# Attention and a feed-forward layer on one core: how the inverse row sums get from one column to all partitions

## The reference

```python
# q, k, v: (4, 8, 1152, 64) fp32; w_in (512, 2048), w_out (2048, 512), alpha (2048)
q_pool = q.reshape(B, H, S // 2, 2, D).mean(axis=3)            # 576 queries per head
scores = scale * np.matmul(q_pool, k.transpose(0, 1, 3, 2))
scores = scores - np.max(scores, axis=-1, keepdims=True)
attn = np.exp(scores)
attn = attn / (np.sum(attn, axis=-1, keepdims=True) + 1e-09)
attn_out = np.matmul(attn, v)
x = attn_out.transpose(0, 2, 1, 3).reshape(2304, 512)
h = x @ w_in
g = np.maximum(h, 0.0) + alpha * np.minimum(h, 0.0)
return g @ w_out
```

## Time and profile before

| | |
|---|---|
| median of three runs | 931.14 us (930.97 to 931.58) |
| profiled execution, own time | 932.26 us |
| its span, first to last instruction | 929.7 us |
| TensorE busy | 95% of the span |
| VectorE busy | 56% |
| ScalarE busy | 46% |
| GpSimd busy | 23% |
| mean granted TensorE clock | 0.998 of full speed |
| one row maximum (L432) | 1348 ns |
| one long exponential (L348) | 1112 ns |
| one copy of slot 1 (L465) | 692 ns |

### The profile page before, as it was taken

How to read it: one execution, slowest core, us unless ns; L and a number is a source line. 1 busy time by engine, 2 the same in 40 slices (tenths; PEclk the granted TensorE clock), 3 DMA queues, 4 the chain that set the end, 5 groups by cost and what they waited for, 6 DMA issues and landing times. The chain is left out here.

```text
span 929.7 us, 20770 instructions
## 1 busy us (share of the span) xinstructions
PE 887.3 (95%) x6896; PEld 623.2 (67%) x6896; DVE 516.9 (56%) x836; ACT 423.4 (46%) x963; POOL 213.3 (23%) x182
## 2 busy tenths in 40 slices
PE   3799999999999999999999999999999999999997
PEld 1455555555555555555545799989999999989995
DVE  2676767677767776767676344344444444343442
ACT  2566666666666666666666222222322222322222
POOL 2112111211121112111200323323232323323230
PEclk9999999999999999999999999999999999999999
DMA  7435423542354235523520122212422222322211
GB/s 186 106 83 135 119 65 82 133 121 63 82 133 123 60 82 133 127 57 82 133 71 1 59 68 58 67 62 63 136 57 68 57 68 61 132 59 66 65 36 68
DMA packets 36366, 79.57 MB, mean 86 GB/s; under 512 B 5360, under 2 KB 9456, under 8 KB 36336
## 3 DMA queue, kind: packets, MB, share of 16 engines
q1 hardware_dynamic: 33936, 74.48, 31.0%
q10 hardware_dynamic: 2400, 4.72, 1.5%
HBM read 74.46 MB, written 4.72 MB: 85 GB/s over the span
## 5 line engine op out<-in xcount | busy, mean ns | idle before, releaser
L432 DVE TENSOR_REDUCE neg_max<-s_ps 128x1 f32<-128x1152 f32 x144 | 194.1, 1348 | 16.6 <-DVEq L431 16.6
L573 PE MATMUL pv_ps<-pt,v_f 128*64 128x256 f32 (+1 forms) x1152 | 169.0, 414 | 0.0
L532 PE MATMUL s_ps<-k_f,q_f 64*128 64x512 f32 (+1 forms) x640 | 160.2, 626 | 5.2 <-PEq L543 5.2
L348 ACT ACTIVATE e_sb<-s_ps,neg_max 128x1024 f32<-128x1024 f32 x144 | 160.1, 1112 | 0.0
L587 PEld LDWEIGHTS slot_ps<-ident,e_sb 64*128 64x128 f32 x2304 | 86.0, 139 | 82.4 <-issue 82.4
L465 DVE COPY pt<-slot_ps 128x512 f32<-128x512 f32 x144 | 99.6, 692 | 61.3 <-DVEq L464 59.4
L341 ACT ACTIVATE e_sb<-s_ps,neg_max 128x128 f32<-128x128 f32 x144 | 52.9, 367 | 171.5 <-ACTq L340 171.5
L617 PE MATMUL slot_ps<-x_hi,wi_hi 128*128 128x384 f32 x384 | 129.5, 337 | 1.1 <-PEq L613 1.1
L617 PE MATMUL slot_ps<-x_lo,wi_hi 128*128 128x384 f32 x384 | 129.5, 337 | 0.0
L617 PE MATMUL slot_ps<-x_hi,wi_lo 128*128 128x384 f32 x384 | 129.0, 336 | 0.0
L479 DVE TENSOR_SCALAR e_sb<-slot_ps,alpha_sb 128x384 f32<-128x384 f32 x96 | 59.3, 618 | 123.2 <-DVEq L477 123.2
(11 more groups left out here) (46 smaller groups left out, 1098.8 us busy)
## 6 DMA issues: line engine op xcount, KB each, us to landing
q_raw<-in_q SPq DMA_DIRECT2D x64, 288.0 KB, 4.5
k_f<-in_k SPq DMA_DIRECT2D x64, 288.0 KB, 4.2
wi_raw<-in_w_in SPq DMA_DIRECT2D x48, 256.0 KB, 2.6
wo_raw<-in_w_out SPq DMA_DIRECT2D x48, 256.0 KB, 2.6
v_f<-in_v SPq DMA_DIRECT2D x32, 288.0 KB, 3.0
out<-pt ACTq DMA_DIRECT2D x6, 768.0 KB, 4.4
k_end<-in_k SPq DMA_DIRECT2D x64, 32.0 KB, 4.0
alpha_sb<-in_alpha SPq DMA_DIRECT2D x1, 8.0 KB, 4.7
```

What stands on the lines that cost most here:

```text
L348: nc.scalar.activation(e_sb[:, b * NKEY + at:b * NKEY + at + n], s_ps[:, S_AT[b] + at:S_AT[b] + at + n], ACT.Exp, bias=neg_max[:, b:b + 1] ...
L432: nc.vector.tensor_reduce(out=neg_max[:, b:b + 1], in_=s_ps[:, S_AT[b]:S_AT[b] + NKEY], op=ALU.max, axis=AX_X, negate=True).then_inc(max_r ...
L532: ins = nc.tensor.matmul(s_ps[to:to + m, S_AT[b] + at:S_AT[b] + at + BANK], q_f[2 * g + h][rows, first:first + m], k_f[2 * g + h][rows, at ...
L573: ins = nc.tensor.matmul(pv_ps[h * D:(h + 1) * D, 0:n], v_f[2 * g + h][:, a, :], pt[:, a, at:at + n], start=(a == 0), stop=(a == KT - 1))
```

## The change

The matmuls of `spread_inverse` and ScalarE's copies into `inv_bc` go, on all engines; so do the waits for slot 0 in steps t = 6 and t = 1. Instead SP writes each column of inverses to a row `sums` in DRAM, 128 single elements per DMA (64 for the halves of the mixed tile): six stores for group 0, four for group 1. It waits until all have landed and reads the row back twice, once per head, broadcast to 64 partitions of `inv_bc`. `inv_bc` has room for both groups now. `scale` waits for the two broadcasts in place of ScalarE's copy. SP's loads are split into q with k, and V, to make room for the spreads in its order: group 0 goes ahead of the V loads, group 1 behind the second q, and the first weights stand between the last two spreads.

```diff
+            def load_qk_pair(pair, g):
                 load_q(pair * 2)
                 sp.wait_ge(k_free[g], 1).then_inc(k_free[g], -1)
                 load_k(pair * 2, 2 * g), load_k(pair * 2 + 1, 2 * g + 1)
                 load_q(pair * 2 + 1)
+
+            def load_v_pair(pair, g):
                 sp.wait_ge(v_free[g], 1).then_inc(v_free[g], -1)
                 load_v(pair * 2, 2 * g), load_v(pair * 2 + 1, 2 * g + 1)
+
+            def spread(group):
+                a, b = GROUP_TILES[group]
+                at, other, n, first = GROUPS[group]
+                whole = [t for t in range(a, b) if t != MIX]
+                sp.wait_ge(inv_ready, 1).then_inc(inv_ready, -1)
+                for i in range(0, len(whole), 2):
+                    for h in range(2):
+                        to = GROUPS[group][h] + i // 2 * P
+                        t = whole[i + h]
+                        sp.dma_start(sums[to:to + P], inv_sum[:, t:t + 1]).then_inc(inv_stored, 16)
+                if group == 0:
+                    for h in range(2):
+                        to = GROUPS[group][h] + 2 * P
+                        sp.dma_start(sums[to:to + HALF],
+                                     inv_sum[h * HALF:(h + 1) * HALF, MIX:MIX + 1]).then_inc(inv_stored, 16)
+                stores = len(whole) + (2 if group == 0 else 0)
+                sp.wait_ge(inv_stored, 16 * stores).then_inc(inv_stored, -16 * stores)
+                for h in range(2):
+                    row = sums[GROUPS[group][h]:GROUPS[group][h] + n]
+                    sp.dma_start(inv_bc[h * D:(h + 1) * D, first:first + n],
+                                 row.rearrange("(o n) -> o n", o=1).to_broadcast([D, n])).then_inc(inv_bc_in[group], 16)
...
+            spread(0)
+            load_qk_pair(2, 0)
+            spread(1)
+            with sp.Fori(0, NPAIR // 2 - 2) as two:
                 for g in range(2):
-                    load_pair(two * 2 + g, g)
+                    spread(0)
+                    load_v_pair(two * 2 + 2 + g, g)
+                    load_qk_pair(two * 2 + 3 + g, 1 - g)
+                    spread(1)
+            spread(0)
+            load_v_pair(NPAIR - 2, 0)
+            load_qk_pair(NPAIR - 1, 1)
+            spread(1)
+            spread(0)
+            load_v_pair(NPAIR - 1, 1)
+            spread(1)
+            spread(0)
             load_wi(0, 0, False), load_wi(1, 1, False)
             load_wo(0, 0, False), load_wo(1, 1, False)
+            spread(1)
...
-                if t in SPREAD and (t == 6 or pair is not None):
-                    n = GROUPS[SPREAD[t]][2]
-                    act.wait_ge(spread_ready, 2).then_inc(spread_ready, -2)
-                    nc.scalar.activation(inv_bc[:, 0:n], slot_ps[0][:, 0:n], ACT.Copy).then_inc(act_self, 1)
...
-                dve.wait_ge(inv_bc_ready, 1).then_inc(inv_bc_ready, -1)
+                dve.wait_ge(inv_bc_in[group], 32).then_inc(inv_bc_in[group], -32)
                 dve.wait_ge(pv_done, 2).then_inc(pv_done, -2)
-                nc.vector.tensor_tensor(x_sb[:, first:first + n], pv_ps[:, 0:n], inv_bc[:, 0:n],
+                nc.vector.tensor_tensor(x_sb[:, first:first + n], pv_ps[:, 0:n], inv_bc[:, first:first + n],
...
-                    if t in SPREAD:
-                        pe.wait_ge(slot_free[0], 1).then_inc(slot_free[0], -1)
-                        spread_inverse(SPREAD[t], slot_ps[0])
                     product(group, g if group == 0 else 1 - g, tiles)
...
-            product(1, 1, (0, 1))
-            spread_inverse(1, tail_ps)
-            product(1, 1, range(2, KT))
+            product(1, 1, range(KT))
```

More of the change, by code:

```diff
@@ L13, with build @@
 BANK = 512
-def build(nc, q, k, v, w_in, w_out, alpha, out):
+def build(nc, q, k, v, w_in, w_out, alpha, sums, out):
     HEADS, D, NKEY = k.shape
@@ L49, in build @@
                0: (1, (0, 1)), 1: (1, (2, 3)), 2: (1, (4, 5)), 3: (1, (6, 7)), 4: (1, (8,))}
-    SPREAD = {6: 0, 1: 1}
     INVERT = {4: 0, 8: 1}
@@ L81, in build @@
         inv_sum = sb("inv_sum", [P, TILES])
-        inv_bc = sb("inv_bc", [P, 320])
+        inv_bc = sb("inv_bc", [P, NQ])
         x_sb = sb("x_sb", [P, NQ])
@@ L111, in build @@
                 [s_ps[:, 3 * BANK:4 * BANK], s_ps[:, 4 * BANK:5 * BANK], pv_ps[:, :]]]
-        tail_ps = s_ps[:, 3 * BANK:3 * BANK + 256]
         k_in = [sem(f"k{i}_in") for i in range(4)]
@@ L138, in build @@
         inv_ready = sem("inv_ready")
-        spread_ready = sem("spread_ready")
-        inv_bc_ready = sem("inv_bc_ready")
+        inv_stored = sem("inv_stored")
+        inv_bc_in = [sem(f"inv_bc{i}_in") for i in range(2)]
         pv_done = sem("pv_done")
@@ L216, in load_v @@
                 sp.dma_start(v_f[i][:, :, :], v[head, :, :, :]).then_inc(v_in[i // 2], 16)
-            def load_pair(pair, g):
+            def load_qk_pair(pair, g):
                 load_q(pair * 2)
@@ L242, in _ @@
             sp.dma_start(alpha_sb[:, :], alpha).then_inc(alpha_in, 16)
-            with sp.Fori(1, NPAIR // 2) as two:
+            spread(0)
+            load_qk_pair(2, 0)
+            spread(1)
+            with sp.Fori(0, NPAIR // 2 - 2) as two:
                 for g in range(2):
-                    load_pair(two * 2 + g, g)
+                    spread(0)
[10 more added lines that the diff above has]
+            spread(0)
             load_wi(0, 0, False), load_wi(1, 1, False)
             load_wo(0, 0, False), load_wo(1, 1, False)
+            spread(1)
             for n in range(PASSES):
@@ L359, in step @@
                     exponential(s + 1)
-                if t in SPREAD and (t == 6 or pair is not None):
-                    n = GROUPS[SPREAD[t]][2]
-                    act.wait_ge(spread_ready, 2).then_inc(spread_ready, -2)
-                    nc.scalar.activation(inv_bc[:, 0:n], slot_ps[0][:, 0:n], ACT.Copy).then_inc(act_self, 1)
-                    act.wait_ge(act_self, 1).then_inc(act_self, -1)
-                    act.sem_inc(inv_bc_ready, 1)
-                    act.sem_inc(slot_free[0], 1)
                 if t == TILES - 2:
@@ L395, in _ @@
             wi_high(0), wi_high(1), wo_high(0)
-            act.wait_ge(spread_ready, 2).then_inc(spread_ready, -2)
-            nc.scalar.activation(inv_bc[:, 0:GROUPS[1][2]], tail_ps, ACT.Copy).then_inc(inv_bc_ready, 1)
             for n in range(PASSES):
@@ L547, in transposed @@
                 return nc.tensor.transpose(to, e_sb[:, at:at + P], ident[:, :])
[L549 to L562, removed]
             def product(group, g, tiles):
@@ L701 @@
         args.append(nc.dram_tensor(f"in_{name}", a.shape, mybir.dt.from_np(a.dtype), kind="ExternalInput").ap())
+    args.append(nc.dram_tensor("sums", (S,), F32, kind="Internal").ap())
     args.append(nc.dram_tensor("out", (B * S // 2, DM), F32, kind="ExternalOutput").ap())
```

## The result

The changed kernel takes 977.38 us in the median of 4 runs (975.64 to 986.96), against 931.2 us before: 1.0516 times as long, with a 95% interval of 1.0447 to 1.0585. I had forecast 915.6 with a range of 908.8 to 922.0. The prediction was wrong, and on the other side.

What follows compares the result with a forecast made beforehand. TensorE, 95% busy, was taken to bound the kernel, with a two-step loop as floor. Savings of 6.0 + 8.7 + 0.4 + 0.44, together 15.5 us, with transfers hidden, gave 916.8 profiled, 915.6 median; range 908.8 to 922.

Steps and rivals of the forecast that it cites:

- The removal: Attention stage: dropping TensorE's spread matmuls saves 15.5 us in all; dropping ScalarE's copies is worth nothing.
- T(0) to T(2): TensorE, from the first transpose of a pair's tile 0 to tile 2's: 6.82 us falls to 6.42, saving 0.40.
- T(5) to T(7): TensorE, from the first transpose of a pair's tile 5 to tile 7's: 7.27 us falls to 6.69, saving 0.58.
- the pair: TensorE's period for one pair of heads, T(2) to T(2): 30.88 us falls to 29.9.
- Rival A: TensorE gets back all of 0.61 + 0.72 us per pair, 20.8 us in all, so 910.3; chance 0.16.
- the loop over two steps: TensorE waits on VectorE's copy and maximum, then ScalarE's exponentials: two steps can't take less than about 6.42 us.
- The failed step: SP's stores into DRAM: landing 2.6 us after issue, at most 4.4, taken from the rows by size.
- The other terms: SP's issues at 0.50 us each, and broadcasts landing in 2.6 us, at most 4.5; nothing added in the likeliest case.
- the ring: Round of waits ending where it began; Rival C bounded the pair from group 0's reciprocal to group 1's landing.
- Rival C: SP's round trip delays VectorE's scaling and becomes the bound: 942 us, 973 with everything at the large end; chance 0.12.
- The weights' first loads: Behind the last pair's spread(0): needed 9.6 us of 12.5 available; cost taken as 0, at most 2 us once.
- The page: Skill page: read-modify-write below 512 B, some 2 us fixed cost; the first would be a cause of Rival C.

## Why the prediction was wrong

*The removal: right.* T(0) to T(2) 6.42 us as forecast, with the idle before T(2); T(5) to T(7) 6.77 against 6.69; the pair 29.97 against 29.90 where the transfers are hidden. The forecast of 915.6 is missed by the fast kernels by 1 us, by the kernel without a spread by 2.8 (0.9 us of that is lost in its first pair, against the kernel with the SBUF row; the rest I can't place). Rival A (full return, 910.3) is out: the loop over two steps is as rigid as read, and 0.3 of the 0.72 us at t = 1 turned into a wait.

*The failed step* is the price of the stores: "A few hundred bytes are nearest to the small end: 2.6." Measured are 6.5 and 7.2 us from the last issue to the landing (7.0 on the mean), beyond my large end of 4.4 too. I took the price by size, from rows whose packets are contiguous and large, and the trace before had no row for writes of single elements. The bound was no bound, because it varied the wrong quantity.

*The other terms held, all but twice.* Issues took 0.49 us (0.50), the six stores 3.1 us (3.0), the broadcasts 1.1 (1.0), and they landed in 2.8 in the median (2.6). But two of them took 8.6 and 9.0, twice my large end of 4.5. In these two pairs T(5) to T(6) is 14.4 and 13.3 us, where it is 3.5 in the kernel with the SBUF row: 20.8 of the 55 us that TensorE is behind that kernel at T(8) of the last pair. So the stores' landing explains the ring of 33.1 us, and a second term, which no run here explains, the two pairs beyond it. It comes with the slow stores, though: none of the kernels with fast ones shows it.

*Rival C was the mechanism,* and with its large end its 973 us is near the 977; but that agreement is partly luck: its landings of broadcasts (4.5) and issues (0.65) were too large and that of the stores too small. It also closed the ring in another place. I let the pair run from the reciprocal to the scaling through VectorE; in the trace SP's own turn of 33.2 us closes it in eleven of fourteen turns, and the way through VectorE in the others. By its timeline above, the turn is 3.1 for the stores of group 0, 6.5 for their landing, 1.3 for the broadcasts, 2.3 for V and q, 8.0 to the second q, 1.2 for that, 1.9 for the stores of group 1, 7.2 for their landing and 1.7 up to the next: 33.2. From 29.9 to 33.7 us for some fourteen pairs are 53 us; 7.6 us more arise behind T(8) of the last pair, where T(8) is at 551.34 (496.24 in the kernel with the SBUF row) and the span ends 62.7 us later than there instead of 55.1.

*The weights' first loads* were priced at 0, at most 2 us: the wait for them grew by 3.6, from the same wrong term. *The clock* was not in the forecast: in five pairs TensorE waits 1.65 to 9.92 us for the product and then runs at 1.2 GHz for a few microseconds, which costs some 2 us each (the piece from the product at 242.47 to the next ninth block takes 4.8 us in place of 2.8).

*The page.* The Trainium skill, DMA: Bandwidth & Descriptors (Specifications), warns of a read-modify-write below 512 B. I gave it no weight in the sum. By the runs size alone isn't it: elements of four bytes that lie 16 bytes or more apart land in 2.0 to 2.4 us, and only neighbours take 7.0. The page gives its fixed cost of about 2 us (Anatomy of one DMA) for DMAs that GpSimd issues, and I carried it over to SP's. Here it fits the spaced and the contiguous stores (1.9 to 2.4 us) and fails for neighbours (7.0).

## What to carry to other kernels

Where something waits for it, don't store a column (one element per partition) side by side into DRAM: gather it into a row in SBUF first and store that in one piece, or space the elements. An operation for which the trace has no row wants its price bounded by what makes it different (here the pattern of its writes), not by its size. And where one queue both waits and issues, add up its whole turn and compare that with the period of the bounding engine; a reordering can bring the wait back behind other data in the queue.

## What the runs showed of the hardware that I had not expected

- 128 stores of four bytes that are neighbours in DRAM land in about 7 us, with the DMA queue's packets at 7.0% of the 16 engines; at 8, 16 and 64 bytes apart it is 3.7, 2.4 and 2.0 us on the mean. The same gather into one partition of SBUF takes 1.9 us on the mean.
- A contiguous store of 1 or 1.3 KB into DRAM had landed 0.93 us after its issue ended and 1.44 after it began, faster than the transfers in the earlier trace rows (2.6 us for 256 KB).
- In two turns of the changed kernel a broadcast took 8.6 and 9.0 us to land, where between them the others took 2.4 to 3.6. The cause is open.
- Idles of TensorE of 1.65, 4.00, 4.78, 8.85 and 9.92 us were each followed by some microseconds at half the clock; one of 2.26 us (before the product at 340.01) and those of the earlier trace rows were not.
